# Fused attention and two feed-forward layers: another way to pool q, k and v in the opening, and another order of loads and weights

## The reference

```python
def _attn_ref(q, k, v):                      # (4, 8, 576, 64) each
    q_d = q.reshape(B, H, Sd, 4, D).mean(axis=3)   # Sd = 144; k_d, v_d alike
    out_d = sm_attn(q_d, k_d, v_d)                 # full softmax attention, 144 x 144
    out_up = np.repeat(out_d, 4, axis=2)
    mask = np.abs(pos[:, None] - pos[None, :]) < 4 # local attention, 7 keys a query
    ...
    return out_up + out_local
x = attn.transpose(0, 2, 1, 3).reshape(2304, 512)
xn = x / sqrt(mean(x * x) + 1e-6) * rms_g
y = (silu(xn @ w_gate) * (xn @ w_val)) @ w_out      # 512 -> 1536 -> 512
r = maximum(y @ w_in, 0); out = (s * (r * r) + b) @ w2_out   # 512 -> 2048 -> 512
```

## Time and profile before

| what | value |
|---|---|
| median of three runs | 1050.22 us |
| the profiled execution | 1050.09 us, its span 1048.3 us |
| PE busy | 965.3 us (92%) |
| DVE, ACT, POOL busy | 557.7, 332.3, 393.4 us |
| first gate matmul of chunk 0 | 164.19 us |
| first u of chunk 1 (the silu; one step makes one u) | 231.86 us |
| first gate matmul of chunk 2 | 286.60 us |

### The profile page before, as it was taken

How to read it: one execution, slowest core, us unless ns; L and a number is a source line. 1 busy time by engine, 2 the same in 40 slices (tenths; PEclk the granted TensorE clock), 3 DMA queues, 4 the chain that set the end, 5 groups by cost and what they waited for, 6 DMA issues and landing times.

```text
span 1048.3 us, 13187 instructions
## 1 busy us (share of the span) xinstructions
PE 965.3 (92%) x5056; PEld 783.4 (75%) x5080; DVE 557.7 (53%) x814; ACT 332.3 (32%) x722; POOL 393.4 (38%) x198
## 2 busy tenths in 40 slices
PE   3657787799899999999999999999999999999997
PEld 2545566799877767777777799887888888888896
DVE  6868966877566567556453132334443343343343
ACT  2333446222431243232324154322222232222222
POOL 3647754889387668646550055300000000000000
PEclk9999999899999999999999999999999999999999
DMA  9977443413132222201101333201100200010010
GB/s 242 261 188 190 136 128 108 122 51 118 36 116 73 66 78 91 70 10 40 64 19 42 120 115 119 69 1 41 41 1 1 80 1 1 21 41 1 1 41 21
DMA packets 54639, 77.65 MB, mean 74 GB/s; under 512 B 6224, under 2 KB 37936, under 8 KB 53680
## 3 DMA queue, kind: packets, MB, share of 16 engines
q1 hardware_dynamic: 52560, 72.09, 23.2%
q10 hardware_dynamic: 2016, 4.72, 1.2%
HBM read 66.17 MB, written 10.62 MB: 73 GB/s over the span
## 4 chain that ended last, share of the span: by engine, by line
PE 77%; DVE 7%; DMA 5%; POOL 5%; issue 4%; ACT 1%; SPq 1%; DVEq 0%; ACTq 0%; POOLq 0%
PE bank L609 25%; PE bank L717 6%; PE bank L718 6%; PE bank L719 6%; PE bank L735 6%; PE bank L736 6%; PE bank L737 6%; PE bank L632 4%; PE bank L630 4%; PE bank L631 4%; DMA rawv<-in_v_dram 3%; DVE dv L1105 2%; POOL prod L419 2%; DVE sc L439 1%; DMA ks<-in_k_dram 1%
## 5 line engine op out<-in xcount | busy, mean ns | idle before, releaser
L419 POOL TENSOR_TENSOR prod<-qs,ks 128x896 f32<-128x896 f32 x80 | 174.1, 2198 | 107.8 <-DVE sc L439 70.9
L433 POOL TENSOR_TENSOR prod<-sc,vs 128x896 f32<-128x896 f32 x80 | 150.0, 1978 | 67.2 <-DVE x L449 39.1
L756 DVE SCALAR_TENSOR_TENSOR r<-bank,r 128x512 f32<-128x512 f32 (+1 forms) x80 | 51.1, 638 | 183.8 <-ACT r L744 183.8
L719 PE MATMUL bank<-y_h,w2i_l 128*128 128x512 f32 (+1 forms) x320 | 117.7, 368 | 0.0
L651 DVE TENSOR_TENSOR bank<-bank,u 128x256 f32<-128x256 f32 (+1 forms) x72 | 40.6, 564 | 139.3 <-PE bank L609 130.8
L630 PE MATMUL bank<-h_h,wo_h 128*128 128x256 f32 (+1 forms) x288 | 107.4, 373 | 0.0
L609 PE MATMUL bank<-x_h,wv_h 128*128 128x256 f32 (+1 forms) x288 | 103.1, 374 | 1.6 <-DVE h_l L657 1.6
L744 ACT ACTIVATE r<-bank 128x512 f32<-128x512 f32 (+1 forms) x80 | 44.4, 555 | 183.8 <-PE bank L719 183.1
L609 PE MATMUL bank<-x_h,wg_h 128*128 128x256 f32 (+1 forms) x288 | 92.6, 346 | 7.0 <-ACT u L639 6.9
L632 PE MATMUL bank<-h_h,wo_l 128*128 128x256 f32 (+1 forms) x288 | 97.9, 340 | 0.0
L631 PE MATMUL bank<-h_l,wo_h 128*128 128x256 f32 (+1 forms) x288 | 97.2, 337 | 0.0
(11 more groups left out here) (118 smaller groups left out, 1966.5 us busy)
## 6 DMA issues: line engine op xcount, KB each, us to landing
raww<-in_moe_w_out_dram SPq DMA_DIRECT2D x14, 512.0 KB, 3.9
rawq<-in_q_dram SPq DMA_DIRECT2D x4, 1152.0 KB, 8.9
rawk<-in_k_dram SPq DMA_DIRECT2D x4, 1152.0 KB, 11.0
rawv<-in_v_dram SPq DMA_DIRECT2D x4, 1152.0 KB
ks<-in_k_dram SPq DMA_DIRECT2D x16, 280.0 KB
vs<-in_v_dram SPq DMA_DIRECT2D x16, 280.0 KB
raww<-in_moe_w_in_dram SPq DMA_DIRECT2D x8, 512.0 KB, 3.5
y_raw<-y_scr SPq DMA_DIRECT2D x4, 1024.0 KB, 4.8
```

The costliest lines, as they stand in the source:

```text
L419: pool.tensor_tensor(dst, qv, kv, ALU.mult).then_inc(prod_ready, 1)
L433: pool.tensor_tensor(dst, pv, vv, ALU.mult).then_inc(prod_ready, 1)
L719: last = pe.matmul(o, w2i_l[:, m, kk, :], y_h[t % 2][:, kk, 0:w], start=False, stop=kk == DT - 1)
```

## The change

q is summed by PE itself: raw rows of one head are the stationary operand (72 groups by 128 values, which are two of the four tokens), and a constant `neg` (the identity times minus the scale) is the moving one; two matmuls accumulate, and the result, in 128 partitions, holds two half sums. The score matmul adds them up by contracting over 128 partitions, for which ACT copies the transposed k twice, into both halves of the partitions. Half of v's rows are summed by PE too (four matmuls of 512 columns with the identity), the other half by DVE. All sums of k are now on POOL. A batch has eight units on PE (`UNIT`), placed by `POOL_SLOT`. Queries and rows of v are split between even and odd groups rather than first and second half. The last batch works on the norm of tile 0 earlier. SP's list of loads is new; weights come in the order in which the first chunk uses them (`FIRST_ORDER`), and only two pieces are split before the first chunk. The other 16 are split during chunk 0 (`HI_AT`, `LO_AT`, six of them on POOL between products of tile 1). Reductions of tile 1 have new places (`QK1_AT`, `PV1_AT`), with the softmax of tile 1 in steps 11 of chunk 0 and 0 of chunk 1, and its rounds of transposes in steps 9 to 11 of chunk 1.

```diff
+UNIT = [("q", 0), ("k", 0), ("q", 1), ("k", 1), ("q", 2), ("k", 2), ("q", 3), ("v", 0)]
+POOL_SLOT = {5: (0,), 6: (1, 2), 7: (3,), 8: (4, 5), 9: (6,)}
+FIRST_ORDER = [("gate", 0), ("val", 0)]
+for _j in range(1, M1 // 2):
+    FIRST_ORDER += [("gate", _j), ("val", _j), ("out", _j - 1)]
...
+QK1_AT = {1: (4,), 2: (5,), 3: (6,), 4: (7, 8), 5: (9,), 6: (10, 11), 7: (12,), 8: (13,), 9: (14,), 10: (15,)}
...
-            for g in range(6):
-                transpose_pooled(0, g)
+                if kind == "q":
+                    for c in range(4):
+                        h, a = 2 * g + c // 2, c % 2
+                        for f in range(2):
+                            col = (2 * a + f) * 2 * D
+                            last = pe.matmul(o[:, c * JH:(c + 1) * JH], rawq[0:JH, h, col:col + 2 * D], neg[0:JH, :], start=f == 0, stop=f == 1)
+                elif kind == "k":
+                    for t in range(3):
+                        last = pe.transpose(o[0:D, t * P:(t + 1) * P], kd[:, 3 * g + t, :], ident[:, :])
+                else:
+                    for f in range(FAC):
+                        last = pe.matmul(o[0:JH, :], ident[0:JH, 0:JH], over(rawv[0:JH, 0, (FAC + f) * D:], [[2 * FAC * D, H], [1, D]]),
+                                         start=f == 0, stop=f == FAC - 1)
...
+                    act.activation(kT[0:D, b % 2, cols], CTR[n % 2][0:D, 0:3 * P], ACT.Copy)
+                    act.activation(kT[D:2 * D, b % 2, cols], CTR[n % 2][0:D, 0:3 * P], ACT.Copy).then_inc(ctr_evac, 1)
...
-                    if b + 1 < B:
-                        if 1 <= h < 4:
-                            pool_q(b + 1, h - 1, 3)
-                        if 3 <= h < 7:
-                            pool_v(b + 1, h - 3, 4)
+                    if h in (1, 2):
+                        pool_v(b, h - 1)
...
+            for n in range(4):
+                qk_mult(pool, 1, n)
+            weight_lo(pool, 2)
+            weight_lo(pool, 3)
+            for n in range(4, 16):
+                if n in (6, 9, 12, 14):
+                    weight_lo(pool, {6: 6, 9: 9, 12: 12, 14: 15}[n])
...
+                if c == 1:
+                    if m == 0:
+                        for n in range(4):
+                            qk_reduce(dve, 2, n)
+                        softmax_norm(dve, 1)
+                    for n in PV1_AT.get(m, ()):
+                        pv_reduce(dve, 1, n)
```

More of the change, by code:

```diff
@@ L184, in build @@
         cpT = place(at, "cpT", [P, 2, 2 * J], F32)
-        co = place(at, "co", [P, 2, E], F32)
+        neg = place(at, "neg", [P, JH], F32)
         assert at[0] <= rest_end
@@ L999, in _ @@
             split_bf(act, 0, 1)
-            weight_hi(act, M1)
-            squares0(act, 1)
+            for n in range(2, 5):
+                weight_hi(act, n)
             for s in range(STEPS1):
@@ L1008, in _ @@
                     split_bf(act, c + 1, 1)
-                if c == 0 and m == 0:
-                    weight_hi(act, M1 + 1)
-                    weight_hi(act, M1 + 2)
-                if c == 0 and m == 1:
-                    weight_hi(act, M1 + 3)
+                if c == 1 and m == 0:
+                    softmax_exp(act, 1)
+                if c == 1 and m == 6:
+                    squares(act, 1, 0)
+                if c == 1 and m == 8:
+                    squares(act, 1, 1)
+                if c == 1 and m == 9:
+                    normalise(act, range(FAC), 3)
                 if 2 <= c < NCH - 1:
@@ L1034, in _ @@
                     normalise(act, (2, 3), 2)
-                if c == 0 and m in (1, 2):
-                    weight_hi(act, M1 + 3 + m)
+                if c == 0:
+                    for n in HI_AT.get(m, ()):
+                        weight_hi(act, n)
                 if c == 0 and m in (4, 5):
@@ L1308, in _ @@
                         last.then_inc(cpv, 1)
-                    if h >= 4 and b + 1 < B:
-                        transpose_pooled(b + 1, h - 4)
+                    if h == 1:
+                        pool_unit(b, UNITS - 1)
+                    if b + 1 < B:
+                        for i in POOL_SLOT.get(h, ()):
+                            pool_unit(b + 1, i)
                     if b == B - 1 and h == H:
```

359 lines of the change are left out of this document (182 added, 177 removed).

## The result

The changed kernel takes 1096.57 us, the median of four runs (1091.49 to 1098.81), against 1050.26: a ratio of 1.0437 [1.0397, 1.0477], slower by 46 us. The forecast was 1066 and its range ended at 1085. The profiled execution took 1098.12 us, its span 1096.3.

The account below looks back on a forecast made before the run. At a slow clock PE would bound the opening, gaining 53.5 us of work and losing at most 48.3 of waits. 1050.1 + 11 (opening) + 5 (chunks 0 and 1) = 1066 us; range 1055 to 1085, 8 in 10 1019 to 1085.

Parts of the forecast that it names:

- the likeliest case: Whole kernel: slow clock with PE bounding the opening, slower at 1066 us; chance 0.48.
- slow clock: Opening: PE runs at 1.2 GHz throughout, although the page prints a full clock (1.00).
- PE bound: Opening: PE's work grows from 103.0 to 156.5 us and sets the time, 167.3 us without any wait.
- a later division: Chunk 1: tile 1's softmax division waits behind four reductions, about 11.5 us in; chunk 1 takes 66 us.
- other waits: Opening: of 48.3 us of waits before, 8 stay, between 4 and 20.
- T0: First gate of chunk 0, where the opening ends: forecast at 175.3 us, 11 us later than before.
- I take 0.13, by the moving columns: Opening, q on PE: 256 instructions at 0.13 us each, 33.3 us; at 0.22 it would be 56.3.
- A gain is excluded: Opening, scores: contracting over 128 partitions instead of 64 changes nothing; 32 heads stay at 2.73 us, 87.4 us.
- the pieces and the loads: Chunk 0: weight pieces 2 and 3 and a load behind bring step 2 to about 16 us after the first gate.
- clock up and down: Rival, opening: v's units raise the clock, it falls where PE starves; 1046 us, chance 0.17.
- Fast clock: Rival, opening: mostly 2.4 GHz, POOL bounds, chunk 0 starts at about 132; 1023 us, chance 0.25.
- in all terms at once: Range: bounds on waits, q's instructions and chunks give 1055 to 1100; upper ends together judged unlikely, so 1055 to 1085.

Follow-up runs that it names:

- e3: The changed kernel with q summed by four matmuls of 64 stationary columns instead of two of 128, and scores over 64 partitions; 1116.02 us.
- e2: The kernel before, with transposed q and k copied into both halves of the partitions and scores contracting over 128; 1050.32 us.
- e1: The changed kernel with both halves of DVE's sum of v placed behind the minima of heads 0 and 1; 1085.84, 1085.72, 1086.82 and 1067.22 us.
- e7: e1 with weight pieces 2 and 3 split sooner, on ACT at heads 8 and 9, on POOL behind two products; 1075.47 us.
- e9: e1 with DVE's first four reductions of tile 1 moved into the last batch and ACT's halves of pieces 2 and 3 sooner; 1073.36 us.
- e14: e9 with the division of tile 1 first in chunk 1 and tile 2's first reductions two a step from step 9; 1067.62 us.
- e11: The changed kernel with tile 2's first four products and reductions moved behind tile 1's products with v, so its division comes first; 1091.06 us.
- e13: The kernel before with one part of the change alone: PE sums the second half of v, DVE the first; 1073.62 us.
- e6: The kernel before with q's sums of batches 1 to 3 moved from DVE to POOL; 1053.81 us.
- e17: e14 with eight filler matmuls behind each of a batch's ten rounds in the opening, 40 times; 1058.23 us.
- e4: The changed kernel with 24 filler matmuls, whose result nothing reads, ahead of each unit of v; 1100.82 us.
- e18: e17 with the loads of v's rows for batches 1 and 3 moved ahead in SP's list; 1064.48 us.
- e5: The changed kernel with the edit of e1 and 24 filler matmuls ahead of each unit of v; 1074.42 us.

## Why the prediction was wrong

The direction of the likeliest case was right, and so were three parts of its mechanism: slow clock, PE bound, a later division. Two steps failed: the price of q's instructions, taken by the moving columns (0.13 us, measured 0.2135), and a wait that I put at nothing, the stop behind v's units (12.8 us). The opening's sum, as forecast and as it came (heads, k, q and v are the number of units times the time of one in the rows above; "other waits" is what remains to 198.7):

| term | forecast | measured | off |
|---|---|---|---|
| start | 9 | 10.9 | +1.9 |
| 32 heads | 87.4 | 76.8 | -10.6 |
| k | 7.8 | 7.8 | 0 |
| q, 256 instructions | 33.3 | 54.7 | +21.4 |
| v | 28.0 | 27.3 | -0.7 |
| transposes of x | 1.8 | 1.8 | 0 |
| stop behind v's units | 0 | 12.8 | +12.8 |
| other waits | 8 | 6.6 | -1.4 |
| T0 | 175.3 | 198.7 | +23.4 |

- The step "I take 0.13, by the moving columns" failed. Of the bounds 0.13 and 0.22 the upper was right, and e3 shows why: 64 stationary columns 0.126, 128 stationary 0.2135. I had chosen by the moving side, although had the only instruction with 128 stationary columns at 0.22. The products with v said it too: 72 stationary and 64 moving columns take (44.93 - 43.98) / 8 = 0.119 us, the time of the transposes of 72 and 72, (43.98 - 43.50) / 4 = 0.12. The Trainium skill, "TensorE: Matmul & The Clock Gate", section "LDWEIGHTS (loading the stationary operand)", gives a load as columns over 1.2 GHz, 107 ns for 128 as an estimate. That such a load would hide behind 72 moving columns was my own step. The traces do not agree with either: at this clock the measured pace, 0.2135 us, is twice that figure, and it did not hide.
- "A gain is excluded" for 128 contracted partitions was false. The gain is 0.33 us a head, in e2 and in the kernel after. I had counted columns and not looked at what lies between instructions of 64 and of 72 partitions. Why there is a gain is not shown: e2 and e3 show only that it goes with the height of the contraction, and e2's rows that it lies where the height changes. This error was worth 10.6 us to the other side, so it hid part of the other two.
- The stop of 12.8 us was nowhere in my sum, though the order of DVE's list showed it. I had written of waits at the start of a batch and not asked what the new unit, 6.8 us long, delays: the minimum of head 2, behind which v's own second half stands. e1 removed it and won 11 us.
- Chunk 0 was forecast at 61.5 us and took 70.0 (first gate to first u of chunk 1; before 67.7): no gain of 5 or 6 but a loss of 2.3. I had seen the pieces and the loads as what makes step 2 late. e7 showed that it is not the pieces, e9 that it is DVE's four reductions: without them chunk 0 takes 63.8 us, most of the forecast gain. In the kernel before, DVE's multiplication of step 0 comes 6.6 us behind T0, in the kernel after 12.9.
- Chunk 1 was right: 66 us were forecast and 67.2 came (first u of chunk 1 to first gate of chunk 2; before 54.7). The division ends 10.6 us into it (forecast 11.5), POOL's products with v take 32.4 (forecast 31). e14, with the division first, shows 5.8 us of the loss to be the late division; it still takes 61.0, and the rest I have not tested.

The sum: 1066.3 + 23.4 (opening) + 9.7 (the two chunks, 137.2 where 127.5 was forecast) - 1.3 (the last stretch) = 1098.1, the profiled execution.

The reading of the clock was right against the page's own 1.00. Of the rivals, "clock up and down" describes what the mended kernels do (e1, e7, e9, e11, e14 in some runs), but not one of four runs of the change itself came near 1046. "Fast clock" needed filler, and then the first gate went to 167 and not to the 132 that I had worked out. The clock was up for most of that opening (0.89 in the mean from 40 to 160 us); a load held PE for 7.26 us, and what else holds it is not shown.

My range ended at 1085 because I had put the upper ends aside "in all terms at once". The bounds that I named were also added up wrongly: 1066 with waits -4 and +12, q's instructions up to +23 and chunks -4 to +5 makes 1058 to 1106, not 1055 to 1100. The result lies inside that. The known bound on q's instructions alone, +21 of its 23 us, was enough to leave the stated range; the stop of 12.8 us was in no bound.

## What to carry to other kernels

When work goes to an engine, price each new instruction by the row that shares its larger side (stationary or moving), and keep the whole range where no row has both. Then walk the list of each engine that serves the new unit and ask what now waits for it, two instructions down. An engine that is idle for a third of a stretch is not free: PE was, and yet 27.3 us of v's units there moved the first gate by 24.7 us (e13). And work taken off one engine has to be followed to where it goes: 13 us moved from DVE to POOL gave nothing here (e6), since DVE then waited for POOL.

## What the runs showed of the hardware

- At the low clock a fp32 instruction with 128 stationary and 72 moving columns takes 0.2135 us (kernel after), with 64 stationary 0.126 (e3). At the high clock a unit of 16 takes 1.74 us, 0.109 each (e17).
- At the low clock the starts of equal fp32 instructions lie 0.120, 0.213, 0.240 and 0.853 us apart when the larger of the two sides has 72, 128, 144 and 512 columns; for 72 and 128 that holds for either side (kernels before and after, e3).
- Scores over 64 partitions between instructions of 72 cost 0.33 us a head more than over 128 (2.73 against 2.40 us, and e2).
- The page's granted clock reads 1.00 from the start until the first change that is recorded (e4: 1.00 up to 43 us, though the instructions ahead of the filler were slow). The same kernel before was printed with a mean of 0.995 and 0.922 in runs of equal time (1050.4 and 1050.6 us).
- A clock that was up fell in or behind waits of PE: 3.14 us in e4, 7.26 in e17, 3.96 in e18, but also behind 1.69 in e5 and 1.16 in e7. Between its rise at 40.8 us and its fall at 51.1 e7 had small fp32 matmuls alone.
- A kernel whose opening does not stop differs from run to run with the clock that it gets: 1061.26 to 1083.47 us in e9, while the seven runs of the kernel before beside it lie within 4.1. In e7 the clock rose 3.4 us behind a unit of v, with no filler at all.
